# Placing the small matmul units of the attention in groups between the dense matmuls: both Z together, each X with half a gram, QS with PU, the three transposes

## What is computed

```python
for t in range(S):                       # q, k, v: (4, 8, 768, 48)
    kt, vt, bt = (k_n[:, :, t], v[:, :, t], beta[:, :, t, None])
    y[:, :, t] = np.einsum('bhd,bhde->bhe', q[:, :, t], state)
    v_old = np.einsum('bhde,bhd->bhe', state, kt)
    state = state + bt[:, :, :, None] * np.einsum('bhd,bhe->bhde', kt, vt - v_old)
...
h = x @ w_in                              # (3072, 384) @ (384, 2048)
g = np.where(pos, h, np.where(neg, 0.0, (h + beta) ** 2 / (4.0 * beta)))
x = g @ w_out                             # (3072, 2048) @ (2048, 384)
...
xn = x / rms * rms_g                      # third stage, 384 -> 1536 -> 384
g = xn @ w_gate
return (silu(g) * (xn @ w_val)) @ w_out
```

## Time and profile before

| | |
|---|---|
| median of three runs | 1081.17 us |
| the profiled execution's own time | 1083.05 us |
| its span | 1081.2 us |
| TensorE matmul busy | 1044.9 us, 97% |
| VectorE busy | 578.8 us, 54% |
| ScalarE busy | 418.7 us, 39% |
| mean granted TensorE clock | 0.988 of full speed |

### The profile page before, as it was taken

How to read it: one execution, slowest core, us unless ns; L and a number is a source line. 1 busy time by engine, 2 the same in 40 slices (tenths; PEclk the granted TensorE clock), 3 DMA queues, 4 the chain that set the end, 5 groups by cost and what they waited for, 6 DMA issues and landing times.

```text
span 1081.2 us, 24182 instructions
## 1 busy us (share of the span) xinstructions
PE 1044.9 (97%) x10828; PEld 849.3 (79%) x10828; DVE 578.8 (54%) x983; ACT 418.7 (39%) x673; POOL 9.6 (1%) x20
## 2 busy tenths in 40 slices
PE   6888999999999999999999999999999999999996
PEld 4566677777777777777778888888888888888885
DVE  5869768858948857873356535323324334333322
ACT  5622444454354454444476643232132232232211
POOL 1000000000000000000000000000000000000000
PEclk9888999999999999999999999999999999999999
DMA  8424002300500320030030230200200200100101
GB/s 248 137 35 114 2 3 60 89 2 31 118 3 3 71 78 3 31 118 2 3 117 29 88 116 2 55 4 1 59 1 1 59 1 1 30 1 1 30 1 29
DMA packets 19031, 48.05 MB, mean 44 GB/s; under 512 B 2448, under 2 KB 9232, under 8 KB 17872
## 3 DMA queue, kind: packets, MB, share of 16 engines
q1 hardware_dynamic: 18928, 46.51, 15.8%
HBM read 37.06 MB, written 9.44 MB: 43 GB/s over the span
## 4 chain that ended last, share of the span: by engine, by line
PE 83%; DVE 13%; issue 3%; ACT 1%; POOL 0%; DVEq 0%; POOLq 0%; ACTq 0%
PE bank L673 21%; PE acc L1229 15%; PE hps L1214 15%; PE acc L692 10%; PE hps L673 7%; PE hps L692 4%; DVE inv L979 3%; DVE outer L975 3%; PE bank L1127 1%; PE bank L1153 1%; DVE g L1046 1%; DVE g1l L1053 1%; PE bank L1116 1%; DVE prob L1021 1%; PE bank L1160 1%
## 5 line engine op out<-in xcount | busy, mean ns | idle before, releaser
L590 ACT ACTIVATE g<-bank 128x512 f32<-128x512 f32 x72 | 43.1, 598 | 257.3 <-PE bank L673 142.6
L1214 PE MATMUL hps<-xh,w1h 128*128 128x512 f32 x288 | 121.8, 423 | 5.1 <-DVE g L1046 5.0
L1229 PE MATMUL acc<-g1h,w2h 128*128 128x512 f32 x288 | 120.2, 417 | 1.7 <-DVE g1l L1053 1.6
L878 ACT ACTIVATE g1h<-g 128x512 fp32r<-128x512 f32 x96 | 60.7, 632 | 157.8 <-DVE g L1046 145.1
L1214 PE MATMUL hps<-xh,w1l 128*128 128x512 f32 x288 | 115.0, 399 | 0.0
L1214 PE MATMUL hps<-xl,w1h 128*128 128x512 f32 x288 | 114.9, 399 | 0.0
L1229 PE MATMUL acc<-g1l,w2h 128*128 128x512 f32 x288 | 114.3, 397 | 0.0
L1229 PE MATMUL acc<-g1h,w2l 128*128 128x512 f32 x288 | 114.0, 396 | 0.0
L1053 DVE TENSOR_TENSOR g1l<-g,g1h 128x512 fp32r<-128x512 f32 x96 | 66.2, 690 | 69.1 <-ACT g1h L878 68.6
L1046 DVE SCALAR_TENSOR_TENSOR g<-hps,g 128x512 f32<-128x512 f32 x96 | 65.7, 685 | 61.6 <-ACT g L872 61.3
L869 ACT ACTIVATE g<-hps,half_c 128x512 f32<-128x512 f32 x96 | 65.6, 683 | 58.3 <-PE hps L1214 58.3
(11 more groups left out here) (196 smaller groups left out, 2033.2 us busy)
## 6 DMA issues: line engine op xcount, KB each, us to landing
kqT<-kq SPq DMA_DIRECT2D x22, 384.0 KB, 6.4
v_in<-v SPq DMA_DIRECT2D x6, 768.0 KB, 4.3
k_in<-k SPq DMA_DIRECT2D x6, 768.0 KB, 5.6
x2d<-x2s SPq DMA_DIRECT2D x18, 256.0 KB, 5.6
x2t<-x2d SPq DMA_DIRECT2D x6, 768.0 KB, 5.6
y<-y_t SPq DMA_DIRECT2D x48, 96.0 KB, 2.2
stage<-w_in SPq DMA_DIRECT2D x4, 768.0 KB, 8.0
stage<-w_out SPq DMA_DIRECT2D x4, 768.0 KB, 10.0
```

Source lines behind the costliest of these rows:

```text
L878: act.activation(g1h[:, f % 2, :], g1[:, f % 2, :], ACT.Copy).then_inc(s_gh, 1)
L1214: last = pe.matmul(hps[f % 2][:, :], wt[:, kk, P * f:P * f + P], xx[:, kk, :], start=(kk == 0 and e == 0), stop=(kk == KD - 1 and e == 2))
L1229: last = pe.matmul(acc[j][:, :], wt[:, f, P * j:P * j + P], gg[:, f % 2, :], start=(f == 0 and e == 0), stop=(f == NF1 - 1 and e == 2))
```

## The change

The small units of bodies 1 to 5 no longer stand one by one. A new list, `chain`, makes groups of them, and each group stands at one place. The places are set: they are rounded down to half a feature block, and then lie behind the h units or behind the o units of a block, never within three units of one kind. The places now begin at the first whole block behind `lead` and end at block 15. The three XT stand together before the last h unit. The inversion of the next chunk begins half a block behind the second GK. GQ stays where it was, and so does XE.

```diff
-def solve(c):
+def chain(c):
 
-    out = [(kind, c, hf) for kind in ("Z", "X") for hf in range(HALVES)]
-    if 0 < c < NSTEP - 1:
-        out += [("GK", c + 1, hf) for hf in range(HALVES)]
+
+    nxt = [[("GK", c + 1, hf)] if 0 < c < NSTEP - 1 else [] for hf in range(HALVES)]
+    out = [[("Z", c, 0), ("Z", c, 1)], [("X", c, 0)] + nxt[0], [("X", c, 1)] + nxt[1]]
+    for hf in range(HALVES):
+        out += [[("KS", c, hf)], [("U", c, hf)], [("QS", c, hf), ("PU", c, hf)], [("KU", c, hf)]]
     return out
...
-LAST = 0.94
+GROUP_AT = 2.99 / NFF
...
-    us = solve(k) + serial(k)
-    begin = None
-    for n, u in enumerate(us):
-        ev.append((lead + (LAST - lead) * n / len(us), u))
-        if u == ("GK", k + 1, HALVES - 1):
-            begin = lead + (LAST - lead) * (n + 1) / len(us)
+    first = math.ceil(NF1 * lead)
+    groups, begin = chain(k), None
+    for n, g in enumerate(groups):
+        at = first + (NF1 - 1 - first) * n / len(groups)
+        at = math.floor(2 * at) / 2 / NF1 + GROUP_AT
+        ev += [(at, u) for u in g]
+        if ("GK", k + 1, HALVES - 1) in g:
+            begin = at + 0.5 / NF1
...
-    tail = {("h0", k - 1, NF1 - 1): 0, ("h1", k - 1, NF1 - 1): 1, ("h", k - 1, NF1 - 1): 2}
...
-        if e in tail:
-            out.append(("XT", k, tail[e]))
+        if e == ("h", k - 1, NF1 - 1):
+            out += [("XT", k, n) for n in range(KD)]
```

More of the change, by code:

```diff
@@ L1 @@
+import math
 from contextlib import ExitStack
@@ L78, in inversion @@
     return out + [(("ft", c, 0), 20), (("xd", c, 0), 21)] + [(("ft", c, n), 20) for n in range(1, TURNS)] + [(("vn", c, 0), 17)]
-def solve(c):
-    out = [(kind, c, hf) for kind in ("Z", "X") for hf in range(HALVES)]
-    if 0 < c < NSTEP - 1:
-        out += [("GK", c + 1, hf) for hf in range(HALVES)]
-    return out
-def serial(c):
-    return [(kind, c, hf) for hf in range(HALVES) for kind in ("KS", "U", "QS", "PU", "KU")]
+def chain(c):
[3 more added lines that the diff above has]
+        out += [[("KS", c, hf)], [("U", c, hf)], [("QS", c, hf), ("PU", c, hf)], [("KU", c, hf)]]
+    return out
 NPIECE = NCHUNK * PIECES
```

## The result

The grouped kernel takes 1086.21 us (median of seven runs, 1083.51 to 1088.07) beside 1081.17 us for the kernel before on the same chip: a ratio of 1.0046, 95% interval 1.0034 to 1.0058. It is slower by about 5 us. The time lies at the upper edge of the range and 4 us above the forecast. The profiled execution took 1087.15 us, its span 1085.4.

The account below looks back on a forecast made before the run. TensorE, busy for 97% of the span, was taken as the bound, waiting mostly for VectorE. Seams -2.6 and waits +3.6 us took 1083.05 to 1084.1 profiled, a median of 1082.2 us; range 1077.8 to 1086.3.

Parts of the forecast that it names:

- slower had 0.35: Chance given to a slower median, beside faster 0.21 and same 0.44.
- two stretches at the lower clock: Clock rival: TensorE partly at 1.2 GHz after long waits, 1.7 us lost; one or two stretches give 1084 to 1086; 0.20.
- waits and seams about even: The forecast case: seams save 2.6 us, waits grow 3.6; median 1080.7 to 1083.7; chance 0.44.
- Seams: TensorE, 33 places fewer: Z pairs 1.5 us, GK behind X 1.4, PU behind QS -0.5, XT 0.2; together 2.6.
- The four places of "What moves": Bodies 2 to 5, VectorE's long pieces ahead of awaited ones: waits of 3.3, 1.2, 2.1 and 1.1 + 0.8 us.
- Waits at U, KS, KU, X, Z counted as none: Small units on TensorE: waits at U, KS or KU counted as none; seeing them would show the forecast wrong.
- the clump for ScalarE: ScalarE takes X and GK out in one 2.4 us clump, relu and square due 2.1 us after; counted at nothing.
- The sum: 1083.05 - 2.6 + 3.6 = 1084.1 us for the profiled execution, so a median of 1082.2.
- two rivals with 0.30 between them: Lower clock (0.20) and instruction stream running dry (0.10), each deciding by itself.
- The instruction rival: TensorE's instruction stream runs dry; three or four groups overrunning by 1 us give a median of 1085.5; chance 0.10.
- nine dense matmuls always follow: Argument against dry instructions: two units (2.2 us) and nine dense matmuls (2.1) take 4.3, against 3.9 for a packet's worth.
- its chain: Body 2, VectorE's added steps: gl, ft, vn and g end at 207.3 against 206.2, a wait of 1.1 us.

Follow-up runs that it names:

- a2: The grouped kernel run again unchanged, for a second profile; 1087.38 us.
- e8: Against e5, only each next inversion begun at the dense unit where the grouped kernel begins it; 1083.59 us.
- e5: Against the kernel before, only the grouping: each group at its first member's old place, inversion beginning where it did; 1078.00 us.
- e1: The grouped kernel, with the next inversion begun at the dense unit where it began before the change; 1084.14 us.
- e7: The grouped kernel, with only the group of X and GK of half 0 in body 3 three dense units later; 1087.18 us.

## Why the prediction was right or wrong, step by step

The range held the time, by 0.1 us, and slower had 0.35. That was luck in part: the upper bound of 1086.3 stood for two stretches at the lower clock, and the profile has one, beside a pause, longer waits and a late X; and the same kernel had a median of 1087.38 us in a2, outside the range. The likeliest case, waits and seams about even, did not come.

- **Seams: right.** 2.4 us measured, 2.6 predicted (Z 0.32 for 0.3, X with GK 0.18 for 0.18, QS with PU -0.06 for -0.05, XT 0.00 for 0.02). The drain that the Trainium skill names (TensorEngine Tiling (Array Packing), Key Properties) agrees with GK's seam at full clock: X with GK gives 0.18 where a pair of Z gives 0.32, so the change of parts costs 0.14 us.
- **The four places of "What moves": right by size, one of them not by cause (cover, below).** Late time is 3.6 us for 3.3 in body 2; without the pause and the clock 1.3 for 1.2 in body 3; 2.2 for 2.1 in body 4; and 2.7 for 1.9 in body 5, its first matmul included, which waited 1.5 us and not 1.1. That makes 9.7 us where the sum had 8.5, and 5.1 before where it had 4.9: the waits grew by 4.6 us and not by 3.6.
- **"Waits at U, KS, KU, X, Z counted as none": wrong for one X.** It cost 0.8 us in body 1. The prediction had counted X and GK as the clump for ScalarE and did not ask what both Z, with X only three dense units behind, do to X.
- **The sum: here the prediction failed.** The forecast holds nothing for the clock and the instruction stream. They are two rivals with 0.30 between them, each by itself. They came together, one behind the other: 1.1 us of pause and 1.4 of clock in one place. That is 2.5 us. The waits give 1.0 more than forecast, the late X 0.8 and the seams 0.2: by the ledger 4.5 us in all, where the median missed the forecast by 4.0. The instruction rival's argument against itself ("nine dense matmuls always follow") was wrong as an argument: what counts is how far a packet begins ahead of the matmul that needs it, not the mean rate. The Trainium skill calls a crossing mostly hidden (Runtime: NRT & Kernel Launch, Instruction fetch mechanics). The trace of the grouped kernel agrees with "mostly": 57 packets began in its five bodies, and one stopped TensorE, for 1.1 us.
- **What was not seen at all: cover.** The change starts the groups at the first whole block behind `lead`, 5 to 11 dense units behind vn instead of 2 or 3. The prediction priced the moved VectorE pieces against fixed deadlines of dense matmuls, and did not ask which small units stand ahead of those deadlines. In body 2 its chain gave 1.1 us for the last wait; it was real, 1.5 us, but e8 has the same VectorE pieces and not the wait. So a part of the 4.6 us came from a cause that the prediction did not have.

The ledger of the difference: 4.6 (waits) + 2.5 (pause and clock) + 0.8 (X) - 2.4 (seams) = 5.5 us, beside 5.2 for the bodies and 5.0 for the medians. By the experiments' medians: the grouping -3.4 us (e5), the later groups alone +6.1 (e1 to e5), the earlier inversion alone +5.6 (e8 to e5), both together +8.2. By bodies 2 to 5 of the profiles, without start and body 1, the same four are -2.4, +4.2, +4.9 and +7.7 us. The two moves alone add up to more than both together (11.7 beside 8.2 by the medians, 9.1 beside 7.7 by the bodies), so the sizes of the parts are not exact; that each alone costs more than the grouping gives holds by both measures.

The best version is e5, 1078.00 us: the grouping with neither of the two moves.

## What to carry to other kernels

Removing a gap from a busy engine pays by what stands at the seam that is left: 0.32 us between two Z, which use the same parts of the array, 0.18 from X to GK, which use others, nothing between transposes, and slightly less than nothing where the second unit waits for the first one's end. Small units also are time for another engine: before one is moved, ask which wait it stands ahead of. A change that bundles a gain of 3 us with a new placing should be tried in parts, since here the placing alone cost twice the gain.

## What the runs showed of the hardware

- **A refill of instructions stops TensorE where it starts too short a time ahead of the matmul that needs it.** In six profiles a pause of 0.8 to 1.9 us stood inside a unit of 64 small matmuls, seven in all, always ahead of matmul 4,526 or 6,176 of the program. The 16 KB packet had begun 0.3 to 1.4 us ahead of the unit and took 1.4 to 1.7 us, where most take 0.9 to 1.2, and TensorE went on 2.8 to 3.2 us behind the packet's start. The unit that began 3.0 us behind its packet (e7) did not stop. A packet close ahead of a small unit is not enough: in bodies 2 to 5 of the 13 profiles one began 0.3 to 1.4 us ahead of 99 other places of small units without such a pause, five of them X with GK behind a packet of 1.5 to 1.7 us.
- **The length of a stop alone doesn't tell whether the clock falls behind it.** In bodies 2 to 5, steps of 1.10 to 1.94 us within small units had a stretch at 1.2 GHz behind them five times of five (one of them a wait for `prob`, in e8); those of 0.83 to 0.95 us, not once in three. Behind steps of 1.3 to 2.1 us between dense matmuls (as at 206.55 and 285.82 us) it never fell, behind a wait of 2.1 us ahead of GQ in two profiles of seven. In body 1, behind a step of 2.5 us between dense matmuls, it fell in 9 profiles of 13.
